# Attention, top-1 experts and a feed-forward block in one kernel: the output transposes and the gate logits of a block in one product

## Chip, cores and metric

The kernel runs on one core of a Trainium2 chip. Its engines are TensorE (PE), VectorE (DVE), ScalarE (ACT), GpSimd (POOL) and SyncE (SP, used here for DMA). The metric is the device time of one execution in microseconds; lower is better.

## What is computed

All data are float32. Three stages follow one another:

```python
# attention: B=2, H=8, S=576, D=64; window of 128 keys, causal, with a linear bias per head
scores = q @ k.T / sqrt(D) - slope[h] * |i - j|      # where 0 <= i - j < 128, else -1e9
attn   = exp(scores - max);  attn /= attn.sum() + 1e-9
x      = (attn @ v)                                  # as 1152 tokens x 512
# experts: E=8, D=512, F=1024, capacity 288, top 1
logits = x @ w_gate;  e = argmax(logits);  gate = softmax(logits)[e]
# token i goes to the next free row of expert e, if there is one
y      = relu(disp[e] @ w1[e]) @ w2[e]
x2     = gate * y                                    # zero for tokens that found no row
# feed-forward, 512 -> 2048 -> 512
h = x2 @ w_in;  out = (h * sigmoid(h)) @ w_out
```

## The kernel before

The 1152 tokens are ten blocks t = 0 to 9 of 128 queries (blocks 4 and 9 have 64). Each block is two half-blocks u = 2t and 2t + 1 of four heads. The five engines run programs of their own that are written out in the order of the work and meet in semaphores.

One turn t of TensorE's loop (lines 1120 to 1154) does, in order: the scores of u = 2t (L1049); the transposes of the probabilities of u - 1 (`turn_p`, L1066); for block t - 2 the transposes of its output (`turn_x`, L1098) and its gate logits (`logits`, L1106); the product with v of u - 2 (`values`, L1089); the transposes of the next q (`turn`, L1033); the scores of 2t + 1; `turn_p` of 2t; the transposes of the next k; `values` of 2t - 1; and the small matmuls that count for block t - 2 how many tokens chose each expert (`places`, L1113, L1114).

`values` leaves the output of a block transposed and not yet divided by the row sums in the PSUM bank bO. ScalarE copies it to SBUF as x_rawT (`take_xT`, L587). `turn_x` transposes it back with the identity into bO: four chunks of 128 columns, each of two heads. `logits` multiplies the same four chunks of x_rawT by the gate's weights (16 columns a chunk, since the two heads have to be kept apart until they are divided) into bank bX. Float32 matmuls that aren't transposes are issued as two passes; a transpose is one. The stationary operand of both is x_rawT; the moving one is the identity or `wg`.

VectorE turns bO into `x_tile` with the reciprocals of the row sums (`normalize`, L779), and the logits likewise (`logits_weigh`, L787), sums the logits over the heads (L794), finds the smallest of their negatives (L799), the expert (L805, L807), the one-hot row (L808) and the running counts (L811). Between these it adds the bias to the scores and takes the row minima (`scores`, L748), and copies half of the turned probabilities (`take_pT`, L760). ScalarE does the exps (L570), the other half of the copies (L581), and the copies of the turned q and k (`take_q` L553, `take_k` L559). GpSimd multiplies x_tile by the gate weight (L498), scatters the rows to DRAM (L506), and splits expert weights into a high part (L476) and a low part (L459) from block 1 to 6.

The tail behind the loop (L1155 to L1170 for TensorE, L870 to L892 for VectorE) handles blocks 8 and 9 in an order written out by hand. The expert plan (L898 to L914) follows. Then all engines take one of two versions of the expert stage.

TensorE fills two waits with products that nobody reads (`keep_busy`, L1179, 128x512): WARM[0] = 6 of them while the plan is made, and WARM[1] = 12 while the dispatched rows come from DRAM. The experts begin with transposes of these rows (`turn_slots`, L1186); the products of the expert stage are L1199 to L1202, those of the feed-forward L1175 to L1177.

Waits that the change touches:

```python
if s == 0 and 1 <= t < NTOK - 1:
    pe.wait_ge(x_ready, t)          # values: bO is free when x_tile is made
...
if t >= 2:
    pe.wait_ge(lg_read, t - 1)      # turn of q: bX is free when the logits are read
```

## Time and profile before

| | us |
|---|---|
| median of 3 runs | 470.28 |
| lowest and highest | 463.39, 472.9 |
| the profiled execution, its time | 465.1 |
| its span, first to last instruction | 463.3 |
| mean granted TensorE clock in it | 0.977 |

The profile is of one execution. Its page gives per engine: TensorE 441.1 us busy (95% of the span), VectorE 231.7, ScalarE 222.1, GpSimd 236.6. The attention blocks run to about 88 us, the routing tail and the plan to 103, the experts from 109 to about 300, the feed-forward from there to the end.

How such lines are read: in the order of time, a line has the start in us from the start of the span, the duration in us, the engine, the line of the kernel, the operation, the tiles written and read, the shape, and the number of instructions that were merged into it. A bracket at the end has the idle time of the engine just before and what ended it. PE is the matmul, PEld the load of its stationary operand. Shapes such as 128*64 128x128 are the stationary operand and the moving one. The granted clock is a share of 2.4 GHz; 0.50 is 1.2 GHz.

### The profile page before, as it was taken

To read this page: it belongs to the slowest core of one execution; us is meant where nothing else is said; L and a number is where in the kernel's file an instruction comes from. 1 tells how busy PE (TensorE), PEld (TensorE's weight loads), DVE (VectorE), ACT (ScalarE), POOL (GpSimd) and SP (SyncE) were. 2 spreads that over 40 slices of the span, in tenths; PEclk is the share of its full clock that TensorE was granted. 3 is DMA by queue.
4 is the path that set the end of the run, shared out by engine and by line. 5 is a ranking of instruction groups with operands and counts; after the bars stand their busy time and mean duration, and the time that the engine had idled before them with its cause. 6 is when DMAs were issued, how large, how long until landed. Compare 5 with 4: busy or idle time off the path is not lost.

```text
span 463.3 us, 8375 instructions
## 1 busy us (share of the span) xinstructions
PE 441.1 (95%) x2939; PEld 400.1 (86%) x2939; DVE 231.7 (50%) x711; ACT 222.1 (48%) x549; POOL 236.6 (51%) x170
## 2 busy tenths in 40 slices
PE   5899999979999999999999999999999999999993
PEld 4677777758999999999999999998999988999982
DVE  4578887766674866857755342132322131312230
ACT  4877778633685666675677643122222221221220
POOL 3006788741989899999999996602000002000002
PEclk9999999858999999999999999999999999999998
DMA  9999960028968697697898500001000001000002
GB/s 177 272 275 254 313 192 12 25 89 288 377 208 262 226 317 256 209 303 282 234 280 301 184 1 1 0 2 45 23 0 0 0 0 68 0 0 0 0 0 74
DMA packets 54567, 64.29 MB, mean 139 GB/s; under 512 B 32096, under 2 KB 32096, under 8 KB 54528
## 3 DMA queue, kind: packets, MB, share of 16 engines
q1 hardware_dynamic: 52752, 59.08, 41.5%
q0 software_dynamic: 1776, 4.73, 2.8%
q8 instruction: 20, 0.33, 0.3%
q14 instruction: 19, 0.16, 0.1%
HBM read 54.35 MB, written 9.44 MB: 138 GB/s over the span
## 4 chain that ended last, share of the span: by engine, by line
PE 79%; DVE 9%; ACT 7%; issue 2%; DMA 1%; POOL 0%; DVEq 0%; POOLq 0%
PE bank L1175 14%; PE bank L1176 14%; PE bank L1177 14%; PE bank L1202 14%; PE bank L1201 6%; PE bank L1049 3%; ACT prob L570 3%; DVE w_lo L971 3%; PE bank L1089 3%; PE bank L1199 3%; PE bank L1066 2%; ACT w_hi L600 2%; PE bank L1033 1%; PE bank L1200 1%; DVE bank L936 1%
## 5 line engine op out<-in xcount | busy, mean ns | idle before, releaser
L459 POOL TENSOR_TENSOR w_lo<-w_raw,w_hi 128x1024 fp32r<-128x1024 f32 x72 | 179.2, 2522 | 22.9 <-ACT w_hi L600 19.6
L1000 DVE TENSOR_TENSOR g_full<-bank,sigmoid 128x384 f32<-128x384 f32 x48 | 26.8, 558 | 131.8 <-ACT sigmoid L686 126.7
L541 POOL DMA_INDIRECT out_dram<-out_stage,permcol x9 | 8.8, 972 | 150.8 <-ACT out_stage L706 147.5
L686 ACT ACTIVATE sigmoid<-bank 128x384 f32<-128x384 f32 x48 | 23.6, 492 | 125.1 <-PE bank L1177 116.4
L600 ACT ACTIVATE w_hi<-w_raw 128x1024 fp32r<-128x1024 f32 x74 | 77.8, 1053 | 0.0
L936 DVE TENSOR_REDUCE bank<-bank 128x192 f32<-128x384 f32 (+5 forms) x96 | 49.1, 512 | 38.4 <-PE bank L1202 38.3
L1175 PE MATMUL bank<-x_hi,w_hi 128*128 x192 | 64.9, 338 | 0.0
L1177 PE MATMUL bank<-x_hi,w_lo 128*128 x192 | 64.6, 336 | 0.0
L1176 PE MATMUL bank<-x_lo,w_hi 128*128 x192 | 64.5, 336 | 0.0
L1202 PE MATMUL bank<-hidden,w_hi 128*128 128x384 f32 (+5 forms) x224 | 63.1, 351 | 0.0
L1175 PE MATMUL bank<-w_hi,g_hi 128*128 128x512 f32 x144 | 56.7, 394 | 0.8 <-DVE g_lo L1004 0.8
L1202 PE MATMUL bank<-xT,w_hi 128*128 128x384 f32 (+5 forms) x192 | 56.7, 351 | 0.0
L1176 PE MATMUL bank<-w_lo,g_hi 128*128 128x512 f32 x144 | 56.5, 392 | 0.0
L1201 PE MATMUL bank<-hidden,w_lo 128*128 128x192 f32 (+5 forms) x224 | 55.6, 248 | 0.7 <-DVE hidden L951 0.6
L1177 PE MATMUL bank<-w_hi,g_lo 128*128 128x512 f32 x144 | 56.1, 389 | 0.0
L1201 PE MATMUL bank<-xT,w_lo 128*128 128x192 f32 (+5 forms) x192 | 48.4, 252 | 0.0
L570 ACT ACTIVATE prob<-prob,neg_max 128x256 f32<-128x256 f32 (+2 forms) x80 | 37.3, 468 | 17.1 <-DVE neg_max L748 17.1
L1201 PEld LDWEIGHTS bank<-hidden,w_lo 128*128 128x128 f32 x224 | 42.7, 191 | 2.0 <-DVE hidden L951 1.9
L1202 PEld LDWEIGHTS bank<-hidden,w_hi 128*128 128x128 f32 x224 | 42.2, 188 | 0.0
L1175 PEld LDWEIGHTS bank<-x_hi,w_hi 128*128 128x128 f32 x192 | 36.1, 188 | 1.7
L1176 PEld LDWEIGHTS bank<-x_lo,w_hi 128*128 128x128 f32 x192 | 36.0, 188 | 1.5
L1201 PEld LDWEIGHTS bank<-xT,w_lo 128*128 128x128 f32 x192 | 36.5, 190 | 0.0
(139 smaller groups left out, 794.3 us busy)
## 6 DMA issues: line engine op xcount, KB each, us to landing
w_raw<-in_moe_w_dram SPq DMA_DIRECT2D x64, 512.0 KB, 5.5
dispatch_dram<-zeros SPq DMA_DIRECT2D x4, 1152.0 KB, 7.7
w_raw<-in_moe_w_in_dram SPq DMA_DIRECT2D x8, 512.0 KB, 5.5
w_raw<-in_moe_w_out_dram SPq DMA_DIRECT2D x8, 512.0 KB, 7.1
dispatched<-dispatch_dram SPq DMA_DIRECT2D x9, 384.0 KB, 8.0
q_raw<-in_q_dram SPq DMA_DIRECT2D x8, 256.0 KB, 5.3
k_raw<-in_k_dram SPq DMA_DIRECT2D x8, 256.0 KB, 5.5
v_raw<-in_v_dram SPq DMA_DIRECT2D x8, 256.0 KB, 5.6
```

Of the source, the lines that this page charges most:

```text
L459: nc.gpsimd.tensor_tensor(wlo[s][:, sl], raw[s][:, sl], whi[s][:, sl], ALU.subtract).then_inc(pool_lo, 1)
L570: nc.scalar.activation(prob[0:r, u % 2, m, c0:c0 + n], prob[0:r, u % 2, m, c0:c0 + n], ACT.Exp, bias=nmin[0:r, t % 2, h:h + 1], scale=-1.0 ...
L600: nc.scalar.activation(whi[s][:, sl], raw[s][:, sl], ACT.Copy).then_inc(whi_ready, 1)
L686: nc.scalar.activation(sig[:, f % 2, :], bank[f % 4][:, 0:TB], ACT.Sigmoid).then_inc(sig_ready, 1)
L936: nc.vector.tensor_reduce(bk[:, 0:w], both, axis=AX.X, op=ALU.add).then_inc(summed, 1)
L971: nc.vector.tensor_tensor(wlo[s][:, sl], raw[s][:, sl], whi[s][:, sl], ALU.subtract).then_inc(dve_lo, 1)
L1000: nc.vector.tensor_tensor(gf[:, f % 2, :], bank[f % 4][:, 0:TB], sig[:, f % 2, :], ALU.mult).then_inc(gf_ready, 1)
L1175: nc.tensor.matmul(dst, ah, bh, start=first, stop=False)
L1176: nc.tensor.matmul(dst, ah, bl, start=False, stop=False)
L1177: return nc.tensor.matmul(dst, al, bh, start=False, stop=last)
L1201: nc.tensor.matmul(dst, al, x[:, 0, 0:w], start=False, stop=False)
L1202: return nc.tensor.matmul(both, ah, x[:, :, 0:w], start=False, stop=last)
```

## The change

The identity and the gate's columns stand side by side in one tile, `comb` [128, 4, 144]: columns 0 to 127 of each chunk are the identity, 128 to 143 the gate's. One product per chunk gives both, 144 columns of which the first 128 are the turned output. GpSimd copies the identity four times into `comb` at the start, and the gate's DMA goes into its last columns. Three chunks (XA = 3, 432 columns) land in bX, the fourth in bS[1][0], a bank of the odd half-block's scores (for block 8 in bO). Normalization and weighing on VectorE are now done in two parts, chunks 0 to 2 and chunk 3, part by part in front of the second scores of the half-block; before, the weighing stood behind them.

TensorE's waits move with it: `values` waits for the copy x_rawT instead of x_tile; the turn of q waits for the first part being read (xa_read); the scores of 2t + 1 wait for both parts (x_ready, lg_read). The product of block t - 2 waits for the places of block t - 3 being read before it starts, where before only the logits did. In the tail, block 8 uses the fused product in front of `turn_p`, and its later `turn_x` is gone; block 9 keeps logits and transposes apart (`last_logits`, `last_turn_x`). WARM goes from (6, 12) to (8, 7).

```diff
-    WARM = (6, 12)
+    WARM = (8, 7)
+    XL = P + 2 * E
+    XA = KC - 1
...
+        def x_at(t):
+
+            a, b = bX, bS[1][0] if t < NTOK - 2 else bO
+            return a[0:ROWS[t], 0:XA * XL].rearrange("p (c x) -> p c x", c=XA), b[0:ROWS[t], 0:XL].unsqueeze(1)
+
+        def split_x(t):
+
+            if t == NTOK - 1:
+                return [(0, KC, out_bank(t)[0:ROWS[t], :].rearrange("p (c x) -> p c x", c=KC),
+                         bS[0][0][0:ROWS[t], 0:H * E].rearrange("p (c x) -> p c x", c=KC))]
+            a, b = x_at(t)
+            return [(0, XA, a[:, :, 0:P], a[:, :, P:]), (XA, KC, b[:, :, 0:P], b[:, :, P:])]
...
-            nc.gpsimd.memset(wg[:], 0.0)
+            nc.gpsimd.memset(comb[:, :, P:], 0.0)
             nc.gpsimd.memset(zeros[:], 0.0).then_inc(zeros_ready, 1)
+            pool.wait_ge(ident_ready, 1)
+            nc.gpsimd.tensor_copy(comb[:, :, 0:P], ident[:].unsqueeze(1).broadcast_to([P, KC, P])).then_inc(comb_ready, 1)
...
+            def normalize(t, part):
+                r, parts = ROWS[t], split_x(t)
+                c0, c1, x, _ = parts[part]
...
+                heads = rrec[0:r, t % 2, 2 * c0:2 * c1].rearrange("p (c h) -> p c h", h=2)
+                ins = nc.vector.tensor_tensor(xt[0:r, t % 4, c0 * P:c1 * P].rearrange("p (c h d) -> p c h d", h=2, d=D),
+                                              x.rearrange("p c (h d) -> p c h d", h=2),
+                                              heads.unsqueeze(3).broadcast_to([r, c1 - c0, 2, D]), ALU.mult)
...
                 if t >= 2:
-                    normalize(t - 2)
+                    for part in range(2):
+                        normalize(t - 2, part)
+                        logits_weigh(t - 2, part)
                 scores(u, 1)
                 if t >= 2:
-                    logits_weigh(t - 2)
                     logits_sum(t - 2)
...
                 if s == 0 and 1 <= t < NTOK - 1:
-                    pe.wait_ge(x_ready, t)
+                    pe.wait_ge(xT_ready, t)
...
             def turn_x(t):
...
+                r = ROWS[t]
+                pe.wait_ge(xT_ready, t + 1)
+                a, b = x_at(t)
+                for c in range(KC):
+                    dst = a[:, c, :] if c < XA else b[:, 0, :]
+                    last = nc.tensor.matmul(dst, xuT[:, t % 2, c, 0:r], comb[:, c, :], start=True, stop=True)
+                last.then_inc(x_turned, 1)
...
                 if t >= 2:
-                    turn_x(t - 2)
+                    pe.wait_ge(qk_ready, 2 * t + 2)
                     if t >= 3:
                         pe.wait_ge(places_read, t - 2)
-                    logits(t - 2)
+                    pe.wait_ge(scores_ready, QUAD * u)
+                    turn_x(t - 2)
                 if t >= 1:
                     values(u - 2)
                 if t + 1 < NTOK:
                     if t >= 2:
-                        pe.wait_ge(lg_read, t - 1)
+                        pe.wait_ge(xa_read, t - 1)
...
+                if t >= 2:
+                    pe.wait_ge(x_ready, t - 1)
+                    pe.wait_ge(lg_read, t - 1)
                 scores(u)
...
             pe.wait_ge(places_read, NTOK - 2)
-            logits(NTOK - 2)
+            turn_x(NTOK - 2)
             turn_p(U - 1)
-            turn_x(NTOK - 2)
             values(U - 1)
-            pe.wait_ge(lg_read, NTOK - 1)
+            pe.wait_ge(scores_ready, QUAD * U)
             places(NTOK - 2)
-
-            logits(NTOK - 1)
-            turn_x(NTOK - 1)
-
-            pe.wait_ge(scores_ready, QUAD * U)
+            last_logits(NTOK - 1)
+            last_turn_x(NTOK - 1)
+            pe.wait_ge(pT_dve, U)
             places(NTOK - 1)
```

## Rows read from the trace of the kernel before

**Rows 1.** Busy time by stretch; last columns: granted clock, DMA share, GB/s.
```profile
60.00:80.00 20.00, 18.71 (x187) 15.29 (x185) 17.56 (x74) 15.52 (x53) 16.47 (x17) 1.00 0.30 95
...
300.00:400.00 100.00, 99.49 (x502) 89.97 (x501) 26.50 (x52) 24.74 (x54) 5.83 (x6) 1.00 0.05 16
```
**Rows 2.** In order of time, TensorE in blocks 6 and 7.
```profile
55.24 0.60 PE L1098 MATMUL bank<-ident,x_rawT 128*64 128x128 f32 x4
...
63.17 1.09 PE L1066 MATMUL bank<-ident,prob 128*128 128x128 f32 x8
...
64.10 0.60 PE L1098 MATMUL bank<-ident,x_rawT 128*128 128x128 f32 x4
...
64.54 0.96 PE L1106 MATMUL bank<-w_gate_sb,x_rawT 128*128 128x16 f32 x8
...
65.73 1.09 PE L1089 MATMUL bank<-probT,v_raw 128*64 128x128 f32 x16 [0.24 <-issue]
```
**Rows 3.** The same view, VectorE, ScalarE and GpSimd in block 7, and its last small matmul.
```profile
64.91 0.68 DVE L779 TENSOR_TENSOR x_tile<-bank,row_rec 128x512 f32<-128x512 f32 x1
...
65.51 0.41 DVE L748 CUSTOM_DVE_ANT_0 prob<-bank,bias 128x256 f32<-128x256 f32 x1
...
66.19 0.22 DVE L787 TENSOR_TENSOR logits_by_head<-bank,row_rec 128x64 f32<-128x64 f32 x1
...
67.40 1.07 DVE L808 TENSOR_SCALAR onehot<-wdesc,best 128x8 fp32r<-128x8 f32 x1
67.42 1.04 POOL L476 CAST w_hi<-w_raw 128x1024 fp32r<-128x1024 f32 x1
...
68.63 0.42 DVE L748 CUSTOM_DVE_ANT_0 prob<-bank,bias 128x256 f32<-128x256 f32 x1
...
69.10 0.51 ACT L570 ACTIVATE prob<-prob,neg_max 128x256 f32<-128x256 f32 x1 [1.05 <-DVE neg_max L748]
...
70.58 0.58 ACT L559 ACTIVATE kT<-bank 128x512 f32<-128x512 f32 x1
...
71.21 0.27 PE L1113 MATMUL bank<-seen,ones 128*128 128x8 f32 x1 [0.24 <-ACT kT L559]
```
**Rows 4.** The same view, VectorE's first operation of second halves, blocks 2 and 8.
```profile
25.97 0.42 DVE L748 CUSTOM_DVE_ANT_0 prob<-bank,bias 128x256 f32<-128x256 f32 x1 [0.69 <-PE bank L1049]
...
77.61 0.42 DVE L748 CUSTOM_DVE_ANT_0 prob<-bank,bias 128x256 f32<-128x256 f32 x1 [0.23 <-PE bank L1049]
```
**Rows 5.** The same view, VectorE's logits chain in block 9.
```profile
84.72 0.79 DVE L805 SCALAR_TENSOR_TENSOR eqw<-logits_neg,lmin,wdesc 128x8 f32<-128x8 f32 x1
```
**Rows 6.** The same view, VectorE's first scores of the kernel.
```profile
8.75 0.29 DVE L748 CUSTOM_DVE_ANT_0 prob<-bank,bias 128x128 f32<-128x128 f32 x1 [2.71 <-PE bank L1049]
```
**Rows 7.** The same view, from the values of half-block 18 to the last logits.
```profile
88.06 1.12 PE L1089 MATMUL bank<-probT,v_raw 128*64 128x64 f32 x16 [0.56 <-ACT probT L581]
...
89.33 1.15 PE L1106 MATMUL bank<-w_gate_sb,x_rawT 128*128 128x16 f32 x8
...
91.56 0.48 DVE L760 COPY probT<-bank 128x128 f32<-128x128 f32 x2 [0.32 <-PE bank L1066]
...
92.50 1.71 PE L1089 MATMUL bank<-probT,v_raw 128*64 128x64 f32 x16
...
94.69 1.03 PE L1106 MATMUL bank<-w_gate_sb,x_rawT 128*64 128x16 f32 x8
```
**Rows 8.** Busy time from 90.1 to 107.2; then in order of time to the first expert product.
```profile
90.10:107.20 17.10, 14.46 (x64) 10.89 (x64) 8.95 (x49) 5.44 (x12) 7.30 (x9) 0.50 0.28 89
...
102.90 4.98 PE L1182 MATMUL bank<-w_hi 128*128 128x512 f32 x12 [2.10 <-issue]
...
106.32 1.95 SPq L323 DMA_DIRECT2D w_raw<-in_moe_w_dram  x4
...
107.72 0.82 PE L1186 MATMUL bank<-ident,dispatched 96*128 96x96 f32 x8
...
109.02 0.41 PE L1199 MATMUL bank<-xT,w_hi 128*128 128x384 f32 x1 [0.48 <-DVE xT L941]
```

More of the change, by code:

```diff
@@ L231, in out_bank @@
             return bO if t < NTOK - 1 else bS[0][1]
[L233 to L235 removed]
+        def x_at(t):
[7 more added lines that the diff above has]
+            return [(0, XA, a[:, :, 0:P], a[:, :, P:]), (XA, KC, b[:, :, 0:P], b[:, :, P:])]
         def places_at(t):
[L239 removed]
+            return (bX if t < NTOK - 2 else bS[1][1] if t == NTOK - 2 else bP[1])[:, 0:E]
         def halves(t):
@@ L783, in logits_weigh @@
-            def logits_weigh(t):
-                r = ROWS[t]
-                dve.wait_ge(lg_done, t + 1)
-                settle()
-                nc.vector.tensor_tensor(lgh[0:r], logits_at(t).rearrange("p (h e) -> p h e", h=H),
-                                        rrec[0:r, t % 2, :].unsqueeze(2).broadcast_to([r, H, E]), ALU.mult).then_inc(lg_read, 1)
+            def normalize(t, part):
+                r, parts = ROWS[t], split_x(t)
+                c0, c1, x, _ = parts[part]
+                if part == 0:
+                    dve.wait_ge(x_turned, t + 1)
+                    if t >= 4:
+                        dve.wait_ge(gated, t - 3)
+                    settle()
+                heads = rrec[0:r, t % 2, 2 * c0:2 * c1].rearrange("p (c h) -> p c h", h=2)
+                ins = nc.vector.tensor_tensor(xt[0:r, t % 4, c0 * P:c1 * P].rearrange("p (c h d) -> p c h d", h=2, d=D),
+                                              x.rearrange("p c (h d) -> p c h d", h=2),
+                                              heads.unsqueeze(3).broadcast_to([r, c1 - c0, 2, D]), ALU.mult)
+                if part == len(parts) - 1:
+                    ins.then_inc(x_ready, 1)
@@ new lines, in logits_weigh @@
+            def logits_weigh(t, part):
+                r, parts = ROWS[t], split_x(t)
+                c0, c1, _, lg = parts[part]
+                if part == 0:
+                    if t == NTOK - 1:
+                        dve.wait_ge(lg_done, 1)
+                    else:
+                        dve.wait_ge(x_turned, t + 1)
+                    settle()
+                heads = rrec[0:r, t % 2, 2 * c0:2 * c1].rearrange("p (c h) -> p c h", h=2)
+                nc.vector.tensor_tensor(lgh[0:r, 2 * c0:2 * c1].rearrange("p (c h) e -> p c h e", h=2),
+                                        lg.rearrange("p c (h e) -> p c h e", h=2),
+                                        heads.unsqueeze(3).broadcast_to([r, c1 - c0, 2, E]),
+                                        ALU.mult).then_inc(lg_read if part == len(parts) - 1 else xa_read, 1)
@@ L877, in _ @@
             slot_base(NTOK - 2)
-            normalize(NTOK - 2)
+            normalize(NTOK - 2, 0)
+            normalize(NTOK - 2, 1)
             sums_guarded(NTOK - 1)
@@ L1096, in turn_x, with last_logits, last_turn_x @@
                 pe.wait_ge(xT_ready, t + 1)
+                a, b = x_at(t)
                 for c in range(KC):
-                    last = nc.tensor.transpose(out_bank(t)[0:r, c * P:(c + 1) * P], xuT[:, t % 2, c, 0:r], ident[:])
+                    dst = a[:, c, :] if c < XA else b[:, 0, :]
+                    last = nc.tensor.matmul(dst, xuT[:, t % 2, c, 0:r], comb[:, c, :], start=True, stop=True)
                 last.then_inc(x_turned, 1)
-            def logits(t):
-                r = ROWS[t]
+            def last_logits(t):
                 pe.wait_ge(xT_ready, t + 1)
-                at_t = logits_at(t)
                 for c in range(KC):
-                    last = nc.tensor.matmul(at_t[:, c * 2 * E:(c + 1) * 2 * E], xuT[:, t % 2, c, 0:r], wg[:, c, :], start=True, stop=True)
+                    last = nc.tensor.matmul(bS[0][0][0:ROWS[t], c * 2 * E:(c + 1) * 2 * E], xuT[:, t % 2, c, 0:ROWS[t]],
+                                            comb[:, c, P:], start=True, stop=True)
                 last.then_inc(lg_done, 1)
+            def last_turn_x(t):
+                for c in range(KC):
+                    last = nc.tensor.transpose(out_bank(t)[0:ROWS[t], c * P:(c + 1) * P], xuT[:, t % 2, c, 0:ROWS[t]], ident[:])
+                last.then_inc(x_turned, 1)
             def places(t):
```

25 lines of the change are left out of this document (8 added, 17 removed).

## Prediction

> **What bounds the kernel now.** I read the table by stage first. From the experts on, TensorE is busy for 99.49 of 100 us at the full clock [rows 1]: whatever moves the start of the experts moves the end by as much, and nothing else of this change reaches it. The attention blocks before that look similar (18.71 of 20 us), but a busy share says little of short passes that wait on one another, so I read block 7 in order of time. Its end is not set by TensorE. ScalarE's copy of kT ends at 71.16, and the matmul that waits for it starts at 71.21 [rows 3]; the next block's scores follow it. In all seven blocks that turn an output and copy a next kT (t = 2 to 8) that matmul starts 0.05 to 0.10 us behind the copy; one of the seven stands in the rows. ScalarE comes to that copy through the exps of the block's second half, which wait for VectorE's second set of row minima. So a block's length is fixed by **when VectorE starts the scores of the second half** (68.63 in block 7, behind the one-hot chain [rows 3]), and some 2.5 us are added after it. VectorE either waited there for TensorE (five times, 0.69, 0.35, 0.55, 0.42 and 0.23 us in blocks 2, 3, 5, 6 and 8, of which [rows 4] has the first and the last) or came late from its own work (blocks 4, 7 and 9, no wait). That wait is the slack with which the change has to be paid.
>
> **The terms.** Times are those of the profiled execution: span 463.3, 465.1 with what lies around it.
>
> *TensorE, per block.* Removed: four transposes and eight gate passes. Eight transposes last 1.09 and four 0.60, so 0.12 per pass of 128 columns [rows 2]; the gate passes (16 columns, 128-wide weights) 0.96 for eight, about 0.11 each, set by their weight load. Added: four products of 144 columns, in float32 two passes each: eight passes. In block 6, where the weights have 64 columns, four transposes took the same 0.60 [rows 2], so I take the moving columns as the measure: 0.12 to 0.135 each, about 1.0 us against 1.3 to 1.35. From below, nothing under the 0.11 of the weight load; from above, load and columns one after the other, 0.11 + 0.12 = 0.23, or 1.8 us. I take 0.12, because eight transposes in a row hide their loads. TensorE gives back 0.3 us. It also loses the wait of the values for x_tile (0.24 [rows 2]), since the out bank is free once x_rawT is copied. So TensorE reaches the second scores 0.4 to 0.6 us earlier, except in block 6, where the values wait for ScalarE's probT.
>
> *VectorE, per block.* x_turned is signalled behind the eighth pass, not the fourth: 7 x 0.125 - 3 x 0.12 = 0.52, call it 0.54. In most blocks VectorE was still copying probT when the transposes ended, so the normalization starts only 0.36 later (0.54 in 5 and 6, where it waited). It is now two instructions, and so is the weighing. 512 elements take 0.68 and 64 take 0.22 [rows 3], so 0.15 plus 1.03 ns an element: 384, 48, 128 and 16 take 0.55, 0.20, 0.28 and 0.17. Each overlaps the next by 0.08 (64.91 + 0.68 against 65.51), so the scores of the first half's second part start 0.90 behind the normalization instead of 0.60: 0.66 later in all. That is hidden: ScalarE, which waits for them, idles for 1.05 before its next exps at 69.10 [rows 3]. The weighing that stood behind those scores (0.25) is gone, so the logits chain is late by 0.36 + 0.30 - 0.25 = 0.41, by 0.59 in blocks 5 and 6.
>
> *A rule that speaks against the split:* the Trainium skill, VectorE: DVE Perf Modes, "The TRN2 errata — SBUF-src ops pay a fixed extra latency per instruction", says that several small tiles each pay the fixed part, some 150 cycles. By it two more instructions cost 0.31 a block, where the overlap leaves me 0.05 net; over eight blocks that would add 2 us to the sum.
>
> *VectorE's late start against its slack [rows 4].* Block 2: 0.34 - 0.69, a gain of 0.35 (TensorE is earlier by 0.44). Block 3: +0.06. Block 5: +0.04. Block 6: +0.15. GpSimd's cast adds a step: in block 7 the 128x8 one-hot took 1.07 and ended with the cast (67.42 + 1.04), where it otherwise takes 0.23; block 4 looks alike, and in block 9 the operation before it took 0.79 for 0.22 [rows 5]. Block 9 therefore absorbs its 0.41: 0. Block 8: +0.06. Block 4: its first operation would fall into the cast too, +0.64. Block 7: between 0 and 0.64 by which operation meets the cast, +0.2. Sum **+0.8 us**, between -0.4 and +2.0.
>
> *New waits on TensorE.* The q transposes wait for the first part weighed, 0.66 behind the normalization's start (64.91 + 0.36): 65.9 in block 7. TensorE is there at 66.1, with the passes from 64.10 taking 1.0 and the values 1.0. Queued behind are the second scores, turned probabilities and k. The second scores wait for both parts, 66.2; TensorE, four transposes later, arrives at 66.7. Price 0; with the cover gone, a few tenths, below the slack of VectorE's chain. The wait for places read moves ahead of the turning and was met. SyncE's queue is untouched.
>
> *Start.* GpSimd makes one more copy, 128x512. GpSimd's cast of twice the elements took 1.04 [rows 3]; I bound the copy by half and by one and a half of that, and in the worst case VectorE's bias stands still as long; VectorE then waits 2.71 for the first scores [rows 6]. Cost 0.
>
> *Routing tail.* Logits (8) and transposes (8) were on either side of turned probabilities, the first from 89.33. Fused, about 1.0 stands for 1.08, and about 1 us of half-clock transposes leaves the path to the values. Those started at 92.50; VectorE's last probT copies end at 92.04 [rows 7]. They bind next: **-0.45**, carried through the last block. Then +0.35 together.
>
> *In front of the experts.* The dispatched rows are there at 106.32, but the twelve unread products (4.98 in all, about 0.43 each at half clock) hold TensorE, whose slot transposes start at 107.72; the first product follows at 109.02 [rows 8]. With seven, 3.0 us from 103.3, the products end at 106.4 and the rows come at 106.67: they are late next. Transposes from 106.7, first product 1.3 later plus 0.2 for two transposes at half clock: 108.2, **-0.8** against 109.02, the +0.35 included. The two more before the plan end at 101.4 to 101.7, before TensorE is released at 102.9: 0.
>
> **Sum: -0.8 us, 464.3** for this execution. It ran 5.2 below the median (470.28). The four executions shown (463.39, 465.1, 470.28, 472.9) have the mean 467.9, and I count from that: **467**.
>
> **Rivals,** each from 467.9.
> - **The clock is late for the experts.** The granted clock is 0.50 (1.2 GHz of 2.4) from 90.1 to 107.2 and rises while the twelve products run [rows 8], 1.8 us before the first product that counts. After seven and a gap it may rise later, in the experts' own passes; counted from the first slot transpose as the trace has it from the restart, 102.9 to 107.2, it comes at 111.0, 2.8 behind the first product at 108.2, and half of that is lost, 1.4. It decides from the point at which the rise comes behind 108.2; 467.9 - 0.8 + 1.4 = 468.5, slower than before. For: less work in one piece. Against: the slot transposes follow almost at once. 0.2.
> - **VectorE's delay is not covered,** because TensorE does not arrive earlier: the delays without slack are 0.34 + 0.41 + 0.64 + 0.59 + 0.57 + 0.41 + 0.29 = 3.25 instead of 0.8, 469.6. 0.15.
> - **TensorE sets the blocks after all:** 0.3 + 0.24 in eight blocks, -4.3, and none of the +0.8: 462.0. Against it stands the kT copy at each block's end. 0.1.
> - **The clock holds through the tail.** Wider products replace the 16-column ones from 89.33 on. At the full clock the same values took 1.12 at 88.06, against 1.71 at 92.50; the last logits' 1.03 would halve, and the four small ones between would save 0.2: -1.3 with the -0.8, 465.8. The trace shows only that the clock fell while those narrow passes ran [rows 7, 8]. The Trainium skill, TensorE: Matmul & The Clock Gate, "Part 4: PE-mode transpose", says that transposes do not count as work for the clock; by that rule the fused product would count where the transposes did not. The trace has the clock full in blocks in which transposes stand among the products [rows 1], and no row that tells their shares apart. 0.15.
> - My forecast: 0.4.
>
> **Range and chances.** 461.5 to 473: the low end takes in TensorE setting the pace, the high end the uncovered delay with the upper bound of the passes in part, and both the 9.5 us by which executions of one kernel differ here. Two per cent is 9.4 us, about what runs of this kernel can tell from no change. None of the cases moves the time that far; only the spread beside the third rival (0.05) and beside the first two (0.04) does.
>
> **What would show it.** Eight passes with 144 columns, 0.12 apart; values right behind them without waiting for x_tile; VectorE starting the second half's scores with no wait, and about 0.1 us later per block on average; the kT copy still ahead of each block's last small matmul; values of the last half-block at 92.0 plus the shift; slot transposes right behind the rows' arrival. I am wrong if the passes are 0.2 apart, if blocks shorten by 0.5 us each, or if the clock is at 0.50 in the experts.

## The result: 0.75% slower, and the profile after

Over 22 runs each, the new kernel has a median of 469.11 us and the kernel before 465.46. The ratio of comparable executions is **1.0075, with a 95% interval of 1.005 to 1.01**: about 3.5 us slower, against the -0.8 of the forecast. That is within 2% of no change, but on the other side of it than forecast. The kernel has a second, slower state, and the ratio leaves out the executions in it: five of the kernel before, 471.73 to 476.69, and none of the new one. The first traced execution took 470.07 (span 468.3), two later ones 469.27 and 466.92.

The attention blocks are bounded by what the prediction's trace reading said. In order of time, block 7 of the new kernel (start, duration, then what ended the idle time before it):
```profile
64.36 1.15 PE L1130 MATMUL bank<-ident_w_gate,x_rawT 128*128 128x144 f32 x8
...
65.44 1.09 PE L1118 MATMUL bank<-probT,v_raw 128*64 128x128 f32 x16
...
65.55 0.56 DVE L796 TENSOR_TENSOR x_tile<-bank,row_rec 128x384 f32<-128x384 f32 x1 [0.29 <-PE bank L1130]
...
66.02 0.20 DVE L812 TENSOR_TENSOR logits_by_head<-bank,row_rec 128x48 f32<-128x48 f32 x1
66.14 0.28 DVE L796 TENSOR_TENSOR x_tile<-bank,row_rec 128x128 f32<-128x128 f32 x1
66.33 0.16 DVE L812 TENSOR_TENSOR logits_by_head<-bank,row_rec 128x16 f32<-128x16 f32 x1
...
66.42 0.41 DVE L762 CUSTOM_DVE_ANT_0 prob<-bank,bias 128x256 f32<-128x256 f32 x1
...
66.87 0.51 ACT L584 ACTIVATE prob<-prob,neg_max 128x256 f32<-128x256 f32 x1 [1.28 <-DVE neg_max L762]
...
67.05 1.14 PE L1079 MATMUL bank<-kT,qT 64*128 64x256 f32 x8
...
68.91 0.42 DVE L762 CUSTOM_DVE_ANT_0 prob<-bank,bias 128x256 f32<-128x256 f32 x1
...
70.85 0.58 ACT L573 ACTIVATE kT<-bank 128x512 f32<-128x512 f32 x1
...
71.48 0.27 PE L1149 MATMUL bank<-seen,ones 128*128 128x8 f32 x1 [0.81 <-ACT kT L573]
```
Eight fused passes take 1.15, as against 0.60 + 0.96 for the two groups of before [rows 2]. TensorE's second scores come 4.68 us behind the block's first (62.37), against 5.25 before (62.10 to 67.35). But the kT copy still releases the last small matmul, now after an idle 0.81 on TensorE where it was 0.24 [rows 3]: the first half became 0.57 shorter and the second 0.57 longer (4.75 for 4.18).

The tail and the front of the experts answer to [rows 7, 8]. First block 9's second scores and what follows from them, then the fused product of the last whole block, the unread products, and the rows of the first expert:
```profile
84.33 0.34 DVE L762 CUSTOM_DVE_ANT_0 prob<-bank,bias 64x192 f32<-64x192 f32 x1
...
85.36 0.70 DVE L832 SCALAR_TENSOR_TENSOR eqw<-logits_neg,lmin,wdesc 128x8 f32<-128x8 f32 x1
...
88.61 1.12 PE L1118 MATMUL bank<-probT,v_raw 128*64 128x64 f32 x16 [1.07 <-ACT probT L595]
...
89.88 1.33 PE L1130 MATMUL bank<-ident_w_gate,x_rawT 128*128 128x144 f32 x8
...
92.92 0.89 PE L1118 MATMUL bank<-probT,v_raw 128*64 128x64 f32 x8 [0.66 <-DVE probT L774]
...
103.06 0.34 SPq L357 DMA_DIRECT2D dispatched<-dispatch_dram  x1
...
103.22 1.88 PE L1219 MATMUL bank<-w_hi 128*128 128x512 f32 x7 [1.53 <-issue]
...
107.48 1.16 PE L1223 MATMUL bank<-ident,dispatched 96*128 96x96 f32 x8 [2.38 <-DMA dispatched<-dispatch_dram]
107.60 1.95 SPq L335 DMA_DIRECT2D w_raw<-in_moe_w_dram  x4
...
108.83 0.66 PE L1236 MATMUL bank<-xT,w_hi 128*128 128x384 f32 x1 [0.20 <-DVE xT L971]
```
The same stretch by busy time; the column behind the five engines is the granted clock:
```profile
90.00:101.00 11.00, 9.79 (x55) 7.71 (x56) 8.34 (x48) 4.91 (x13) 5.25 (x8) 0.54 0.19 72
101.00:108.00 7.00, 3.09 (x16) 1.99 (x15) 1.05 (x6) 0.66 (x2) 2.76 (x2) 0.99 0.37 105
108.00:115.00 7.00, 6.80 (x29) 6.54 (x28) 4.59 (x19) 2.61 (x7) 1.17 (x1) 0.52 0.89 328
```
The values of the last half-block stand at 92.92 against 92.50, the first product at 108.83 against 109.02. So by the first product this execution had lost nothing. It lost behind it: the clock was back at 1.00 (2.4 GHz) by 101.1, fell to 0.50 at 107.9, 0.4 into the turning of the rows that came after TensorE had stood still for 2.38, and stayed there until 114.8, inside the first expert. The turning of the second expert's rows came at 120.83, against 118.27 before.

To read more than one execution I cut every trace at the same places: the scores that open block 2, those of block 9, the last count, the landing of the first expert's rows (SyncE's next issue), the turning of the second expert's rows, the first product of the dense layers. From the count to the issue of the rows it is 4.94 to 4.97 in all. In us:

| stage | kernel before, e7, e9 (below) | new kernel, three traces |
|---|---|---|
| block 2 to block 9 | 60.81, 60.83, 60.90 | 60.94, 61.34, 61.36 |
| block 9 to the count | 17.39, 17.33, 17.21 | 17.55, 18.58, 17.91 |
| issue to landing, first rows | 3.68, 3.75, 3.57 | 4.54, 4.88, 4.61 |
| landing to second turning | 11.95, 12.08, 12.14 | 13.23, 13.42, 11.60 |
| second turning to dense layers | 136.31, 136.25, 136.24 | 136.24, 136.25, 136.33 |
| dense layers | 201.18, 201.31, 201.19 | 203.71, 201.32, 201.18 |

From block 2 to the second turning the means are 98.8 and 101.6: **+2.8 us, of which only 0.4 lies in the blocks** that the change is about. Ahead of block 2 the table says nothing, and there the traces differ by luck: block 2 opens at 19.48, 21.52 and 21.62 in the first column and at 19.62, 19.19 and 19.71 in the second; with other counts each kernel has the other place too (e2 19.23, e3 21.66). What decides it wasn't looked for.

These +2.8 are not the whole 3.5. All six traces have a mean granted clock of 0.975 to 0.98. Of all the executions of the kernel before that the experiments' ratios count, 31 of 87 had 0.984 or more, and their mean time is 464.1 us; none of the 22 of the new kernel had. Between 0.975 and 0.982 the means are 465.69 (51 executions, pooled over four chips) and 468.54 (16): +2.85, as the traces have it. The rest comes from those at the higher mean clock and from five of the new kernel below 0.975. No trace caught one at the higher clock, so why the kernel before has them is open.

The odd 203.71 holds one gap, where VectorE's g_lo took 3.02 while GpSimd's w_lo ran:
```profile
260.51 10.04 POOL L473 TENSOR_TENSOR w_lo<-w_raw,w_hi 128x1024 fp32r<-128x1024 f32 x4
...
262.62 3.02 DVE L1034 TENSOR_TENSOR g_lo<-g_full,g_hi 128x384 fp32r<-128x384 f32 x1
...
266.02 0.49 PE L1212 MATMUL bank<-w_hi,g_hi 128*128 128x512 f32 x1 [2.32 <-DVE g_lo L1034]
```

### The profile page after: what moved, and what is told of

Read it like the earlier page. It is cut to its first block, busy times and chain, and to the rows that moved or that the text cites. A ratio compares the mean times of both kernels' runs of the same rounds, so it can differ in the third digit from the quotient of the medians.

```text
span 468.3 us, 8333 instructions
## 1 busy us (share of the span) xinstructions
PE 439.5 (94%) x2900; PEld 397.9 (85%) x2900; DVE 235.2 (50%) x729; ACT 221.8 (47%) x549; POOL 236.3 (50%) x171
## 4 chain that ended last, share of the span: by engine, by line
PE 78%; DVE 10%; ACT 7%; DMA 2%; issue 1%; POOL 0%; SPq 0%; POOLq 0%; DVEq 0%
PE bank L1212 14%; PE bank L1213 14%; PE bank L1239 14%; PE bank L1214 14%; PE bank L1238 7%; PE bank L1079 3%; DVE w_lo L1001 3%; PE bank L1236 3%; PE bank L1096 3%; ACT prob L584 2%; PE bank L1130 2%; PE bank L1118 2%; ACT w_hi L614 2%; PE bank L1237 1%; PE bank L1063 1%
## 5 line engine op out<-in xcount | busy, mean ns | idle before, releaser
L1239 PE MATMUL bank<-xT,w_hi 128*128 128x384 f32 (+5 forms) x192 | 58.5, 360 | 0.0
L1238 PE MATMUL bank<-xT,w_lo 128*128 128x192 f32 (+5 forms) x192 | 49.4, 257 | 0.0
L1238 PEld LDWEIGHTS bank<-xT,w_lo 128*128 128x128 f32 x192 | 37.8, 197 | 0.0
L1239 PEld LDWEIGHTS bank<-xT,w_hi 128*128 128x128 f32 x192 | 37.5, 195 | 0.0
```

The lines of the kernel that those rows point to most:

```text
L1238: nc.tensor.matmul(dst, al, x[:, 0, 0:w], start=False, stop=False)
L1239: return nc.tensor.matmul(both, ah, x[:, :, 0:w], start=False, stop=last)
```

## The experiments

**Which half of the change?** Theory A: the counts of unread products. Theory B: the fused product with VectorE's new order. Four kernels, each the one or the other with other counts:
```
e1: new kernel,        WARM = (6, 12)      e2: kernel before, WARM = (8, 7)
e3: new kernel,        WARM = (8, 12)      e4: kernel before, WARM = (8, 12)
```


> The fused product and the split on VectorE as in the changed kernel, but the unread products as before, 6 and 12. Theory A (the product counts cost the time: with 7 the clock falls to 1.2 GHz in front of the experts and comes back 6 us into them): about +0.4 us against the kernel before, ratio 1.000 to 1.002, and the granted clock is full within the first 2 us of the experts. Theory B (the fused product and VectorE's four instructions cost it): +3 us, ratio 1.006 or more, with either clock. Theory C (a collision of VectorE and GpSimd in the feed-forward block): ratio 1.000 to 1.01 with a TensorE gap of 2 to 3 us behind 257 us in its trace.

> The kernel before with only the unread products changed, 8 and 7. Theory A: most of the loss is here, +2 to +3 us, ratio 1.004 to 1.007, with a stretch at half clock inside the first expert. Theory B: ratio 0.998 to 1.000, a gain of up to 1 us, since seven products are done before the dispatched rows come. Theory C: no fixed loss, ratio near 1.000.

> The changed kernel with 12 instead of 7 unread products behind the plan. Theory A: if 8 products raise the clock before the plan, 12 last about 2.8 us at the full clock and leave 1.5 us of gap instead of 2.6, so the clock should stay full into the experts: ratio 1.000 to 1.002 against the kernel before, 2 to 3 us better than the changed kernel. Theory B: no better than the changed kernel, ratio 1.006 or more.

> The kernel before with 8 instead of 6 unread products ahead of the plan, 12 behind it as before. Theory A: with the clock raised early the 12 products end before the rows come and the experts start up to 1.3 us earlier at the full clock: ratio 0.997 to 1.000. Theory B says the same. If instead the clock falls in the gap before the rows, the ratio is 1.002 to 1.006, which would say that the count ahead of the plan alone does the harm.

Measured: e1 1.0062 (1.0035 to 1.0089), e2 0.9997 (0.9962 to 1.0033), e3 1.0105 (1.0071 to 1.0139), e4 1.0006 (0.9972 to 1.0039). A falls as the main cause: in the kernel before the counts do nothing, and the fused kernels are slow with any of them. In e2's trace the first expert's turning came 1.69 us earlier than in that of before (106.03 for 107.72), and it gave only 0.41 at the second (117.86 for 118.27): TensorE stood still for 0.87 there, since the last of the second expert's rows, which are issued behind 2 MB of weights, landed at 117.73. In the trace of before they had landed at 116.39. Most fused kernels wait there too (0.73 to 1.83 in e1, e3, e5, e8 and e14 to e17), but not the new kernel in its first trace and in e13: there the rows had landed at 119.41 and 120.00, and TensorE, at half clock in the first expert, came for them at 120.83 and 122.35. e1's trace, in order of time:
```profile
121.28 0.69 PE L1223 MATMUL bank<-ident,dispatched 96*128 96x96 f32 x6 [1.57 <-DMA dispatched<-dispatch_dram]
```

**Which part of the fused kernel?** In e5 the last two blocks are as before; in e6 each fused product is taken apart again; e7 moves one wait in the kernel before; e8 moves one instruction of VectorE.
```diff
 e5  values(U - 2); wait places_read
-    turn_x(NTOK - 2)          # fused
+    last_logits(NTOK - 2)
     turn_p(U - 1)
+    last_turn_x(NTOK - 2)
 e6
-    matmul(dst, xuT[c], comb[:, c, :])
+    transpose(dst[:, 0:P], xuT[c], ident)       # four, then
+    matmul(dst[:, P:], xuT[c], comb[:, c, P:])  # four
 e7 (kernel before)
+    pe.wait_ge(places_read, t - 2)
     turn_x(t - 2)
-    pe.wait_ge(places_read, t - 2)
     logits(t - 2)
 e8
     normalize 0; -weigh 0; normalize 1; weigh 1
     scores(u, 1)
+    weigh 0
```


> The new kernel, but the last two blocks (7 and 8) are handled as before: separate gate products, then the turnings behind the turning of the probabilities, one undivided normalization; the loop over the blocks stays fused. With the fused tail as the cause (in the traces so far from block 9's scores to the count: 17.55, 17.91, 18.28 fused, 17.39, 16.63, 17.16 not), it gives back 0.5 to 1 us of the 3.5, a ratio near 1.006. With the whole loss there, 1.000. With the loss in the loop (VectorE's split, the moved wait), it stays at 1.0065 to 1.0085.

> The new kernel with each fused product of 144 columns taken apart into a turning (128 columns, first four) and a gate product (16 columns, four behind them), into the same columns of the same banks and under the same waits, for blocks 0 to 7. VectorE's work and order stay. TensorE's work grows by about 0.3 to 0.5 us a block and VectorE gets its input as much later. If the order, the split on VectorE or the moved wait cost the time, this is as slow as the new kernel or 1 to 3 us slower (1.008 to 1.014). If the 144-column product itself cost it (its effect on the clock or on its neighbours), this comes out faster than the new kernel, 1.000 to 1.004.

> The kernel before, with one wait moved: TensorE waits for the places read by VectorE ahead of the turning of the outputs and not behind it. In the new kernel's trace this wait held TensorE 0.41 us in one block of six. If it is a main cause, 1.002 to 1.005; if it is a minor one, 1.000 (0.4 us is 0.0009).

> The new kernel with VectorE's order changed: both normalizations and the weighing of the last quarter of the gate logits stand before the second scores, the weighing of the first three quarters behind them, as the whole weighing stood before. VectorE's second scores start about 0.2 us earlier than in the new kernel, and TensorE's turning of q waits for VectorE again. If VectorE's late start of the second scores costs the time, 0.2 us in each of six blocks come back, ratio 1.004 to 1.006; if not, it stays at 1.007 to 1.008.

e5: 1.0113 (1.0077 to 1.0149). The fused tail is not the cause. e6: 1.009 (1.0057 to 1.0122), no better, so the 144-column product is not the cost. Its one trace has 66.64 for the blocks, because the clock was at 0.50 from 49.3 to 63.0; where it was full, blocks 2, 3 and 8 are 0.25 longer than in the new kernel (9.23, 9.00 and 9.01, against 8.97, 8.75 and 8.75): the fusing does give time back. e7: 1.0046 (1.0003 to 1.0088), but its trace has the stages of before (60.83, 17.33); inconclusive. The trace shows no price of the moved wait, and the ratio doesn't exclude one. e8: 1.0125 (1.0082 to 1.0168): my expectation fell. The blocks took 63.37, because TensorE's turning of q waits for that weighing (5.1 us in seven waits), and the earlier scores did not pay for it.

**The constant, VectorE's order, the second rows.** e9 builds only the new constant into the kernel before and reads the gate's columns out of it; e10 gives the kernel before VectorE's new order; e11 and e12 issue the second expert's rows earlier, in the kernel before with 8 and 7 and in the new kernel.
```diff
 e10 (kernel before)
-    normalize(t - 2); scores(u, 1); logits_weigh(t - 2)
+    normalize(t - 2, 0, 3); logits_weigh(t - 2, 0, 6)
+    normalize(t - 2, 3, 4); logits_weigh(t - 2, 6, 8); scores(u, 1)
 e11, e12
-    load_w1(expert[1], 2)
+    load_w1(expert[1], 2, range(2))
     sp.wait_ge(step_done, KC)
     load_dispatched(expert[1])
+    load_w1(expert[1], 2, range(2, 4))
```


> The kernel before with only the new constant: the identity with the gate's columns behind it, four times, is built by GpSimd at the start in place of the gate's own tile (2,304 bytes a partition instead of 256, so every later tile lies 2,048 bytes higher), and the gate products read their 16 columns out of it. Turnings, order and VectorE's work are as before. If the loss of the new kernel comes from the copy at the start or from where the tiles lie, 1.005 to 1.008; if it comes from VectorE's work and the order, 1.000 (0.998 to 1.002).

> The kernel before with only VectorE's part changed in the loop: the normalization in two (three quarters, then one), the weighing of the gate logits in two, each right behind its normalization and ahead of the second scores, as in the new kernel. TensorE's products and order are as before. If VectorE's later second scores are the cause, 1.005 to 1.009 (as the new kernel, or more, because the logits come behind the turnings here). If the cause lies with TensorE's new waits or the constant, 1.000 to 1.002.

> The kernel before with the new kernel's 8 and 7 unread products, and with the second expert's rows issued behind two of the four pieces of its first weights, not behind all four. With these counts alone (1.000) TensorE waited 1.22 us for these rows ahead of the second expert's turning. If that transfer bounds the stretch, the turning comes 1.0 to 1.3 us earlier and the ratio is 0.997 to 0.998; if the weights behind it are what comes late next, 1.000.

> The new kernel with the same edit of the issues: the second expert's rows behind two of the four pieces of its first weights. In traces of the fused kernels TensorE reached this turning 12.0 to 13.4 us after the first rows had landed, against 11.7 to 12.1 in those of the kernel before. If this transfer is where the fused kernels lose, 1 to 1.5 us come back and the ratio falls from 1.0075 to about 1.0045 to 1.0055; if the half clock in the first expert or the attention stage holds it, it stays within 0.001 of 1.0075.

e9: 1.0002 (0.9973 to 1.0031); the constant and the moved tiles cost nothing. e10: **1.0067 (1.0041 to 1.0094)**. Its blocks took 63.13 instead of 60.85. In order of time, TensorE and VectorE in its block 7:
```profile
66.44 0.96 PE L1117 MATMUL bank<-w_gate_sb,x_rawT 128*128 128x16 f32 x8
...
68.00 1.09 PE L1100 MATMUL bank<-probT,v_raw 128*64 128x128 f32 x16 [0.59 <-DVE x_tile L781]
...
69.61 1.14 PE L1060 MATMUL bank<-kT,qT 64*128 64x256 f32 x8
```
```profile
66.82 0.55 DVE L781 TENSOR_TENSOR x_tile<-bank,row_rec 128x384 f32<-128x384 f32 x1
67.44 0.21 DVE L791 TENSOR_TENSOR logits_by_head<-bank,row_rec 128x48 f32<-128x48 f32 x1
67.57 0.28 DVE L781 TENSOR_TENSOR x_tile<-bank,row_rec 128x128 f32<-128x128 f32 x1
67.77 0.17 DVE L791 TENSOR_TENSOR logits_by_head<-bank,row_rec 128x16 f32<-128x16 f32 x1
67.85 0.41 DVE L749 CUSTOM_DVE_ANT_0 prob<-bank,bias 128x256 f32<-128x256 f32 x1
```
Here the values wait 0.59 for the last part of x_tile, and the second scores come 5.60 behind the first, against 5.25 before and 4.68 in the new kernel. The new order is a price of 2.3 us over the blocks of e10's trace. In the new kernel the values don't wait for x_tile, and only 0.4 is left. e6 stands between the two: VectorE's new order, TensorE's new waits, no fused product. Over blocks 2, 3, 4, 7 and 8, where its clock was full, e10 is 1.6 us longer than the kernel before, e6 0.4 longer and the new kernel 0.7 shorter. So the waits give back 1.2 there and the fusing 1.1; the new kernel loses in blocks 5 and 6.

e11: 0.9993 (0.9966 to 1.002). The second turning came 10.69 behind the landing instead of 11.72, but the third then 20.30 behind it instead of some 19.6: the weights are late next. e12: 1.0048 (1.0017 to 1.0078); second turning at 10.52, third 19.60 behind it. The 0.0027 between e12 and the new kernel, 1.2 us, are no measure of the second rows alone: the two intervals overlap, and in e12's trace the first rows landed after 3.60, not 4.54 to 4.88, and the clock held through the tail (9 to the count: 16.47). e18 below, with the same edit, gained nothing over e17.

**Is the gap in the dense layers part of it; is it the loop?** e13 and e14 are the new kernel again, e15 is e5 again, one trace each. e16 is e5 with 6 and 12, so that only the loop over the blocks is new.

> The new kernel itself, a second trace. Its first trace had a gap of 2.66 us on TensorE in the dense layers (203.71 us from their first product to the last, against 201.2 in every other trace), behind a VectorE copy that took 3.02 us; without it the sum of its stages comes to about 466.7 us, under the median of 469.1. If that gap is part of what the new kernel loses, it shows again here (203.5 to 204); if it was an accident, 201.2 us, and the time is then 466 to 468.

> The new kernel itself, a third trace, on the same terms: dense layers 203.5 to 204 us if the gap recurs, 201.2 if not. From the landing of the first rows to the turning of the second expert's rows: 12.5 to 13.5 us if that stretch is where the fused kernel loses steadily, 11.7 to 12.1 if it is not.

> The new kernel with the last two blocks handled as before, a second trace (its median of 470.8 is 3.5 us above the time of its first traced execution). If the gap in the dense layers belongs to the kernels with fused products, it shows here in at least one of these looks; if its lateness comes at the start (block 2's scores at 21.5 instead of 19.1) or in the first experts, the time of those stages tells.

> The new kernel with the last two blocks handled as before and with 6 and 12 unread products, so that only the loop over the blocks is new. If the loop's traced time is all of it (about +0.3 us), 1.000 to 1.002. If the loop carries the loss in executions that no trace here has caught, 1.005 to 1.010. If the 8 and 7 products, which let the clock rise early and fall again in the first expert, are a part, this is faster than the same kernel with 8 and 7 (1.0113) by 0.003 or more.

The gap did not come back: dense layers 201.32, 201.18 and 201.28 in e13, e14 and e15, and 201.1 to 201.4 in every other trace. It was one execution's. e16: **1.007 (1.0038 to 1.0103)**: the loop alone carries the loss, though its own traced time is 61.92, 1.1 more than before, and the rest is code that did not change. These traces showed where. Three things:

*Block 9.* Counted from its first scores, VectorE's second scores start at 3.13 in the kernel before and at 3.78 in every trace of the new kernel, e13 to e16 included; everything on VectorE behind them is 0.29 late, and the values of half-block 18 come at 8.06 instead of 7.77. The line of before that answers to 84.33 above:
```profile
83.42 0.34 DVE L748 CUSTOM_DVE_ANT_0 prob<-bank,bias 64x192 f32<-64x192 f32 x1
```
The variants of the kernel before have 7.59 to 7.79, but e2's trace has 8.05 too, with its second scores at 3.13, so a delay of this size isn't the new kernel's alone.

*The clock.* In the kernel before, e7, e9 and e11 the granted clock falls 9.8 to 9.9 us behind those scores, in e2 12.0. The eight gate passes start at 9.0, so that the fall met only the last of them [rows 7]. In the new kernel they start at 9.3, and the clock falls at 10.3 (first trace), 8.6 (e13) and 9.9 (e14). At the full clock the wide passes follow each other by 0.12, at half by 0.24. The new kernel's 1.33 above; the same group in e13, where all eight were met, then in e14, where four were:
```profile
89.92 2.29 PE L1130 MATMUL bank<-ident_w_gate,x_rawT 128*128 128x144 f32 x8
```
```profile
90.40 1.69 PE L1130 MATMUL bank<-ident_w_gate,x_rawT 128*128 128x144 f32 x8
```
In e16, with the same start and a fall at 9.9, the narrow gate passes are met in the same way (0.11, then 0.21), 1.37 for the eight; the wide ones took 1.70 in e1 and 1.73 in e17 with the same start and fall. e16's line, then e1's:
```profile
90.96 1.37 PE L1134 MATMUL bank<-ident_w_gate,x_rawT 128*128 128x16 f32 x8
```
```profile
90.60 1.70 PE L1130 MATMUL bank<-ident_w_gate,x_rawT 128*128 128x144 f32 x8
```
So of the group's 0.55 over the 1.15 of before, 0.2 is the later start and 0.3 the width. The width costs nothing further on: the last values start 12.7 behind block 9's scores in e16, e1 and e17 alike (12.2 in the kernel before), in e16 held by the transposes that the fused kernels don't have there. What is left of the change in the tail is the later start, 0.5 us. When the clock falls is another matter: in e13 it fell 1.1 us earlier than in the kernel before, ahead of the passes, which no delay explains, and in e12, whose attention code is the new kernel's, only at 14.7, behind the last values. What decides that isn't shown.

*A fetch of instructions.* The DMA queues between issue and landing of the first rows, the new kernel first, then e15:
```profile
q1 hardware_dynamic: 320, 0.59, 40.8%
q8 instruction: 1, 0.02, 1.7%
...
dispatched<-dispatch_dram SPq DMA_DIRECT2D x1, 192.0 KB, 4.5
```
```profile
q1 hardware_dynamic: 320, 0.59, 57.3%
...
dispatched<-dispatch_dram SPq DMA_DIRECT2D x1, 192.0 KB, 3.7
```
One packet of 16 KB of program lies among the rows. Over all 20 traces: where it comes 1.1 to 1.8 us behind the issue (six: the new kernel three times, e3, e16, e18), the rows land after 4.54 to 4.88; in the other 14 after 3.57 to 4.08. Where it comes 8 to 11 us behind, among the weights, and the rows are issued as before (five: e1, e5, e8, e15, e17), the second turning comes 12.27 to 13.35 behind the landing, against 11.60 to 12.14 elsewhere, but for the two new-kernel traces whose clock fell in the first expert (13.23, 13.42). In the kernel before it comes 7.9 to 8.9 us ahead of the issue, in all seven traces of it and its variants, and in e6, with the products taken apart, too. The fourteen and the six differ in one more way. The landing of the first part of the rows is signalled in sixteen parts, and the traces have the time of each. In the six traces fifteen parts are there 3.36 to 3.55 behind the issue and the last one 0.98 to 1.19 after them; in the other fourteen the last follows the fifteenth by 0.01 to 0.25. The packet takes 1.1 to 1.8. One part of sixteen held up by about a packet's time is what a packet in the way of it would do, and what a generally slower transfer would not.

The trace doesn't say whose program the packet holds. I took it for TensorE's, because e10, with VectorE's new order alone, leaves it where it was, and TensorE has 1,750 recorded instructions up to the count in the kernel before and 1,695 in the new one. But e12 has TensorE's program of the new kernel, word for word, and differs in the order of SyncE's issues; there the packet comes 8.0 behind the issue, and the rows land after 3.60. So the length of TensorE's program can't be all that places it.

**Can the fetch be moved?** e17 makes TensorE's program 40 instructions longer in front of its first turning (the 82 waits stand in its trace as 40 instructions); e18 adds the edit of e12.
```diff
+    for _ in range(82):
+        pe.wait_ge(ident_ready, 1)
     turn(0, qraw, q_in, bX)
```


> The new kernel with TensorE's program 40 instructions longer: 82 waits on the identity, long met, stand ahead of its first turning, where it waits for q anyway (3.2 us idle there). Nothing else changes. The new kernel's program is 55 recorded instructions shorter up to the last count, and the fetch of TensorE's next 16 KB of instructions, which in traces of the kernel before comes 8 to 9 us ahead of the issue of the first expert's rows, comes 1.2 to 1.8 us behind that issue in the new kernel's three traces; there the rows take 4.5 to 4.9 us to land instead of 3.6 to 4.0. If this meeting costs the time, the fetch is seen 3 to 8 us ahead of the issue here, the rows land in 3.6 to 4.0, the second turning comes 15.4 to 16.2 us behind the issue instead of 16.2 to 18.3, and the ratio falls to 1.003 to 1.0055. If the fetch is only a bystander, 1.0065 to 1.0085.

> The same longer program, with the second expert's rows issued behind two of the four pieces of its first weights (that edit alone brought the new kernel from 1.0075 to 1.0048). If the fetch and the late rows are separate costs, both come back: 1.000 to 1.0025, and the second turning 14.0 to 14.6 us behind the issue of the first rows. If they are one and the same cost, as that edit alone: 1.004 to 1.0055. What neither can give back is VectorE's later start in the last block (0.29 us) and the gate's products met by the half clock (0.2 to 1.0 us).

e17: 1.0082 (1.0045 to 1.0119). e18: 1.0092 (1.0058 to 1.0126). Neither is a test of what it was made for. The added instructions follow each other by 0.106, 4.2 together, and the first turning comes at 6.02 instead of 4.0:
```profile
6.02 1.09 PE L1063 MATMUL bank<-ident,q_raw 128*128 128x128 f32 x4 [6.02 <-issue]
```
The kernel's first scores start at 8.64, where the other traces have 7.01 to 7.65: some 1.5 us, 0.003 of the time, that both ratios may hold (block 2 opens at 21.25 and 20.84, within the 19.1 to 21.7 of the others). e17's trace also has the clock at 0.50 from 123.1 to 126.5, and e18's from 112.0 to 115.4. And the packet did not move: it came 9.23 behind the issue in e17 and 1.22 in e18, the two places it has in the other fused kernels. The landings fit the rule again (3.79, 4.65), and e18's has the one late part (4.49 for 3.51). That the fetch makes the landing late is well supported by this, but no run moved it and nothing else. What decides between the two places stays open; e17 and e18 have the same program on TensorE and one place each.

## Why the prediction was wrong, by its steps

- **What bounds a block:** right. The kT copy ends each block still, and each block became longer or shorter by as much as VectorE's second scores moved in it. The rival in which TensorE sets the blocks is out.
- **The fused passes:** right (0.12 apart, 1.15 for eight, values right behind).
- **VectorE's split:** right. The second part of the first half's scores starts 0.87 behind the normalization (forecast 0.90), and the logits chain 1.55 behind it (1.53 before). By an estimate from the rule of the Trainium skill (VectorE: DVE Perf Modes, "The TRN2 errata — SBUF-src ops pay a fixed extra latency per instruction"), a fixed part of some 150 cycles for each, two more instructions add 0.31. The durations agree with it: 1.20 for the four of block 7, 0.90 for the two of before. The chain does not, at 0.02 more: each of the four starts 0.07 to 0.09 ahead of the end of the one before it.
- **Blocks, +0.8:** measured +0.4 over three traces, +0.13 in the first, in the range given (-0.4 to +2.0). That the sum is near is in part luck. By block (2 to 8) the forecast was -0.35, +0.06, +0.64, +0.04, +0.15, +0.2, +0.06, and the first trace has -0.43, -0.02, -0.23, +0.58, +0.23, +0.01, -0.02. In block 4 one more operation was to meet GpSimd's cast; instead the one-hot, 0.84 before, took 0.23. In block 5 VectorE came late to the first scores (1.39 behind the block's start instead of 0.76), and the moved wait for places, "was met", held TensorE 0.41.
- **Block 9, "0":** wrong, and it is the step that failed first. I let it absorb its 0.41 in GpSimd's cast. In the row of after, that stall was indeed shorter (0.70 for 0.79), but 0.29 of delay stayed. Nothing stands behind the last block to hide it: in e16, with the tail as before, the last values and the count come 0.5 later.
- **Tail, -0.45:** wrong, +0.7 over three traces. The transposes did leave the path to the last values, and those were held by the probT copy as forecast. But the sum took every duration from one execution, in which the clock fell 0.8 us behind the start of the gate passes. It priced 1.0 for a group that starts 0.3 later and takes 1.3 to 2.3 where the half clock meets it; a part of the +0.7 is that the clock fell early in e13 (8.6), which isn't known to be the change's doing. The clock did not hold through the tail (a rival) in any of the three: it fell 8.6 to 10.3 behind block 9's scores, against 9.8 to 12.0 in the kernel before. In e12 it did hold, and the tail took 16.47. The Trainium skill's rule (TensorE: Matmul & The Clock Gate, "Part 4: PE-mode transpose"), that transposes don't count as work for the clock, would have had the wider products help; these rows don't bear it out.
- **Front of the experts, -0.8:** wrong, and the largest miss. The rows were taken to land as in the trace of before. They landed at 107.60, not 106.67, and so the first product came at 108.83, not 108.2: -0.2. Of the 0.93, 0.86 is a longer landing, the same one late part as in e13 and e14. And the sum ended there: I took the first product for the end of what could move. What is gained at the first product meets the second expert's rows 12 us on: in e2 1.69 became 0.41 (ratio 0.9997).
- **The eight products ahead of the plan, "0":** wrong in two of three traces. They brought the clock up at 101.1 and 102.8, it fell again at 107.9 and 109.6 as the first expert began, and from the landing to the second turning it took 13.23 and 13.42, against 11.60 in the third, where the clock rose once, at 108.1.
- **The rival of the late clock** had its effect in these same two traces (0.50 in the experts was my sign of being wrong), by another way than it said: not a rise that came late, but an early one and a second fall. It was priced at 1.4; the stage differs by 1.7.
- **The level:** 467 was counted from 467.9, the mean of four executions, of which two (470.28, 472.9) lie far above the median of 22, 465.46. That the 469.11 measured is only 2.1 from the 467 forecast is luck.

The rival nearest in time, "VectorE's delay is not covered" (469.6), names e10's mechanism (3.25 forecast in the blocks, 2.3 measured), but not the new kernel's: there the delay was covered in the blocks, all but 0.4, and the loss came behind them. Of the 3.5 us, 2.8 have a place: blocks 0.4, tail 0.7, landing of the first rows 1.0, from there to the second turning 0.7. Why the new kernel's program has the fetch among those rows is open.

No version beat the kernel before; the best, e11, is at 0.9993 (0.9966 to 1.002).

## What to carry to other kernels

Where a block's end is set elsewhere, time taken off an engine returns as its idle time, while each delay that came with it stays, and shows in the last block, where nothing follows to hide it. Follow a gain to the next transfer that is as late as the engine, not to the first instruction that starts earlier. And a term priced from one trace near a change of clock has two values: give it both.

## What the runs showed of the hardware

- The same eight passes of 144 columns took 1.22 at the full clock (e12) and 1.33, 1.69 or 2.29, by how many of them the half clock met; eight of 16 columns, met like those of 1.70, took 1.37.
- TensorE's clock rose at 101.1 and fell again at 107.9 after a wait of 2.38 us between short groups, and the first expert ran at half clock for 6.9 us. With twelve unread products and no wait (before, e1, e3, e16) there was no second fall; with seven there was one within 10 us of the landing in the first trace, e5, e6, e13 and e18, a later one in e8 and e17, and none in e2, e11, e12, e14 and e15.
- Waiting instructions whose semaphore has long been met follow each other by 0.106 us on TensorE (e17).
- Packets of the program come in between those of data, and where one of 16 KB lay among the first rows, one of the sixteen parts of the transfer came 1.0 to 1.2 us behind the others: landings of 4.54 to 4.88 with one inside and 3.57 to 4.08 without, in 20 of 20 traces. No run moved the packet alone.
